# Turning both heads' queries at once with DMA copies between partitions, TensorE fillers, and weight splits moved one pair earlier

## The reference

```python
q_pool = q.reshape(B, H, S // 2, 2, D).mean(axis=3)          # B 4, H 8, S 1152, D 64
scores = scale * np.matmul(q_pool, k.transpose(0, 1, 3, 2))
scores = scores - np.max(scores, axis=-1, keepdims=True)
attn = np.exp(scores)
attn = attn / (np.sum(attn, axis=-1, keepdims=True) + 1e-09)
x = np.matmul(attn, v)                                        # then reshaped to 2304 x 512
...
h = x @ w_in                                                  # 512 x 1024
...
x = (ln @ w_out)                                              # 1024 x 512
...
for e in range(E):
    h = np.maximum(x[mask] @ w1[e], 0.0)
    out[mask] = gate_w[mask, None] * (h @ w2[e])
```

## Time and profile before

| | |
|---|---|
| median of three runs | 1127.13 us (1125.83 to 1127.24) |
| the profiled execution | 1129.12 us, of which its span is 1127.4 us |
| TensorE busy in the span | 1088.0 us (97%), 6647 instructions |
| VectorE busy | 750.0 us (67%) |
| ScalarE busy | 612.9 us (54%) |
| GpSimd busy | 381.5 us (34%) |
| attention | about 0 to 553 us |
| dense stage and routing | about 554 to 790 us |

### The profile page before, as it was taken

One profiled execution on the slowest core, in us unless ns is written; L12 is line 12 of the kernel. 1 busy time (PEld: TensorE's weight loads), 2 busy tenths in 40 slices (PEclk: granted clock), 3 DMA queues, 4 the chain that ended last, 5 costly groups with the idle time before them and its releaser, 6 DMA issues.

```text
span 1127.4 us, 20403 instructions
## 1 busy us (share of the span) xinstructions
PE 1088.0 (97%) x6647; PEld 767.4 (68%) x6647; DVE 750.0 (67%) x1632; ACT 612.9 (54%) x1327; POOL 381.5 (34%) x454
## 2 busy tenths in 40 slices
PE   7899999999999999999899999997989999999996
PEld 4565665556656565655588888886768888888885
DVE  4777787777778777777548999898775633333110
ACT  5676666667666666665465434435356534343221
POOL 4545544454554445445322211215112211111101
PEclk8899999999999999999899999999999999999998
DMA  4221122212112221102520000004556653311100
GB/s 129 64 60 36 53 64 64 62 47 56 44 48 65 64 64 46 40 21 77 150 85 19 28 20 19 28 30 185 171 180 239 228 182 113 106 38 49 39 21 1
DMA packets 92705, 85.59 MB, mean 76 GB/s; under 512 B 49006, under 2 KB 69486, under 8 KB 92464
## 3 DMA queue, kind: packets, MB, share of 16 engines
q1 hardware_dynamic: 88592, 72.92, 21.0%
q0 software_dynamic: 4000, 11.28, 3.1%
HBM read 74.73 MB, written 11.27 MB: 76 GB/s over the span
## 4 chain that ended last, share of the span: by engine, by line
PE 44%; DVE 2%; issue 2%; POOL 1%; ACT 1%; DMA 1%; DVEq 0%; ACTq 0%; POOLq 0%
PE h_ps L694 8%; PE h_ps L696 8%; PE h_ps L695 8%; PE o_ps L694 5%; PE o_ps L696 5%; PE o_ps L695 5%; PE t_ps L1170 2%; PE t_ps L1062 1%; PE h_ps L1137 1%; PE h_ps L1186 1%; DVE junk L1266 1%; DMA w_raw_e<-in_moe_w 1%; DVE w_split L1480 0%; POOL x_lo L973 0%; PE h_ps L1084 0%
## 5 line engine op out<-in xcount | busy, mean ns | idle before, releaser
L346 POOL TENSOR_SCALAR probs<-probs,scales 128x576 f32<-128x576 f32 x288 | 209.8, 748 | 263.6 <-DVE scales L547 263.6
L642 ACT ACTIVATE probs<-s_ps,lows 128x576 f32<-128x576 f32 x288 | 211.0, 737 | 146.5 <-DVE lows L518 146.1
L518 DVE TENSOR_REDUCE lows<-s_ps 128x1 f32<-128x576 f32 x288 | 205.2, 753 | 59.1 <-PE s_ps L423 51.3
L371 PEld LDWEIGHTS t_ps<-ident,probs 128*128 128x128 f32 x1152 | 123.8, 141 | 108.4 <-issue 100.4
L423 PE MATMUL s_ps<-kt,qt 64*128 64x288 f32 x1024 | 163.9, 438 | 4.8 <-ACT probs L642 4.8
L371 PE MATMUL t_ps<-ident,probs 128*128 128x128 f32 x1152 | 158.8, 281 | 2.8 <-POOL probs L346 2.0
L472 PE MATMUL pv_ps<-pt,values 128*64 128x512 f32 x576 | 155.2, 618 | 1.0 <-DVE x_t L582 1.0
L556 DVE COPY pt<-t_ps 128x512 f32<-128x512 f32 x144 | 99.4, 690 | 43.7 <-PE t_ps L371 43.6
L423 PEld LDWEIGHTS s_ps<-kt,qt 64*128 64x128 f32 x1024 | 89.3, 190 | 43.4 <-issue 24.5
L992 POOL DMA_INDIRECT out<-junk,target_rows x25 | 29.5, 1182 | 261.0 <-ACT junk L1699 260.7
L637 ACT COPY pt<-t_ps 128x512 f32<-128x512 f32 x144 | 84.4, 586 | 28.5 <-PE t_ps L371 24.5
(11 more groups left out here) (257 smaller groups left out, 2056.2 us busy)
## 6 DMA issues: line engine op xcount, KB each, us to landing
w_raw_e<-in_moe_w SPq DMA_DIRECT2D x60, 512.0 KB, 5.5
k_raw<-in_k SPq DMA_DIRECT2D x32, 256.0 KB, 2.8
q_raw<-in_q SPq DMA_DIRECT2D x32, 256.0 KB, 3.2
token_rows<-x_rows SPq DMA_DIRECT2D x18, 256.0 KB, 2.0
values<-in_v SPq DMA_DIRECT2D x32, 128.0 KB, 2.7
values<-in_v SPq DMA_DIRECT2D x64, 64.0 KB, 2.7
w_raw<-in_moe_w_in SPq DMA_DIRECT2D x4, 512.0 KB, 5.0
w_raw<-in_moe_w_out SPq DMA_DIRECT2D x4, 512.0 KB, 3.8
```

The lines of the kernel that those rows point to most:

```text
L346: nc.gpsimd.tensor_scalar(where, where, scales[:, g % 2, s, c:c + 1], 1.0, ALU.mult, ALU.mult).then_inc(norm_done if c else half_scaled, 1)
L371: last = nc.tensor.transpose(bank[:, i * P:(i + 1) * P], source, ident[:])
L518: nc.vector.tensor_reduce(lows[:, g % 2, s, c:c + 1], s_ps[c][:, :, 0:part], AX.XY, ALU.max, negate=True).then_inc(low_done[c], 1)
L642: nc.scalar.activation(two_halves(probs[g % 2][:, s, :])[:, :, columns(c)], s_ps[c][:, :, 0:part], ACT.Exp, bias=lows[:, g % 2, s, c:c + 1 ...
```

## The change

1. From pair 1 on, GpSimd adds the queries of both heads in one instruction, without `twice`; one turning (piece Q, slot 1) gives both heads, head 0 in partitions 0 to 63 of `qx` and head 1 in 64 to 127; four DMAs copy each half of `qx` into both halves of `qt`. The visit of slot 7 is gone.
2. In step 0 the pieces of pair 1 move from slots 0, 1, 2, 6, 7 to slots 4 to 7. SP loads the keys ahead of the values, and the queries of pair `at + 2` behind the copies.
3. Filler transposes of the identity stand behind every slot of step 0, at the end of attention and at the start of the dense stage; the ones at the program's start change their shapes.
4. `w_in` is loaded in step 14 and its high parts are made in slots 1, 2, 6, 7 of step 15; `w_out`'s are made in slots 4 to 7 of step 16. GpSimd's low parts of `w_in` may start once pair 14 is turned.
5. In slot 1 of step 16 the product stands between the two halves of the turning. The third batch's `merge_scales` of step 0 stands behind slot 8's maxima.
6. The first `x_lo` is made by VectorE (`first_x_lo`).

```diff
-    kq_slots = {0: KA, 1: QA, 2: TAILS, 6: KB, 7: QB}
+    kq_slots = {0: KA, 1: Q, 2: TAILS, 6: KB}
+    first_kq_slots = {4: KA, 5: Q, 6: TAILS, 7: KB}
+    high_slots = (1, 2, 6, 7)
...
+            def move_queries(n):
+                sp.wait_ge(kq_out, kq_count(n, Q))
+                for h in range(2):
+                    first = h * (full + 1)
+                    for u in range(2):
+                        sp.dma_start(qt[n % 2][rows(u), first:first + full, :].rearrange("p t n -> p (t n)"),
+                                     qx[rows(h), :]).then_inc(q_moved, 16)
...
             for at in range(pairs + 1):
+                n = at + 2
+                if n < pairs:
+                    sp.wait_ge(kq_done, kq_count(n - 1, KA))
+                    load_a(n)
                 if at < pairs:
                     if at >= 2:
                         sp.wait_ge(pv_done, key_tiles * (at - 1))
                     load_values(at)
-                n = at + 2
+                if at + 1 < pairs:
+                    move_queries(at + 1)
                 if n < pairs:
-                    sp.wait_ge(kq_done, kq_count(n - 1, KA))
-                    load_a(n)
-                    sp.wait_ge(q_sums, sum_count(n - 1, QA))
-                    load_qa(n)
+                    sp.wait_ge(q_sums, sum_count(n - 1, Q))
+                    load_q(n, 0)
+                    load_q(n, 1)
...
-            add_queries(0, 1)
-            add_queries(1, 0)
+            add_first_queries()
+            add_queries(1)
             add_tail(1)
             for g in range(pairs):
-                if g + 1 < pairs:
-                    add_queries(g + 1, 1)
                 normalise(g, 0)
                 if g + 2 < pairs:
-                    add_queries(g + 2, 0)
+                    add_queries(g + 2)
                     add_tail(g + 2)
                 for b in range(1, len(batches)):
                     normalise(g, b)
+            pool.wait_ge(t_done[1], key_tiles * (pairs - 1))
...
-            for i in range(18):
-                nc.tensor.transpose(s_ps[1][:, 1, 0:P], ident[:], ident[:])
-            for piece, bank in ((KA, t_ps[0]), (QA, t_ps[1]), (TAILS, third_ps)):
+            def warm(bank, times):
+                for i in range(times):
+                    nc.tensor.transpose(bank[:, 0:P], ident[:], ident[:])
...
+            warm(pv_ps, 3)
+            warm_halves(8)
+            warm(pv_ps, 2)
+            warm_quarters(4)
+            warm(pv_ps, 4)
...
+                        warm(pv_ps, 4 if s < 2 or has_kq(at, s) else 8)
                         continue
                     if i is not None:
                         turn_tiles(i, 0)
+                        if at == pairs and s == 1:
+                            multiply(m)
                         turn_tiles(i, 1)
...
+            warm(s_ps[0][:, 0, :], 8)
...
-                    if at == pairs and s > 0:
-                        c = s - 1
+                    if at == pairs - 1 and s in high_slots or at == pairs and in_chunks <= s < w_chunks:
+                        c = s if at == pairs else high_slots.index(s)
...
-                pe.wait_ge(x_lo_done, m + 1)
+                if m == 0:
+                    pe.wait_ge(first_x_lo, 1)
+                else:
+                    pe.wait_ge(x_lo_done, m)
...
+            for i in range(12):
+                nc.tensor.transpose(o_ps[:, 0:P], ident[:], ident[:])
...
+            dve.wait_ge(x_hi_done, 1)
+            nc.vector.tensor_tensor(x_lo[:, 0, :].rearrange("p (b n) -> p b n", n=P), columns_of(x_t, 0),
+                                    x_hi[:, 0, :].rearrange("p (b n) -> p b n", n=P).bitcast(F32),
+                                    ALU.subtract).then_inc(first_x_lo, 1)
```

More of the change, by code:

```diff
@@ L96, in build_attention @@
         k_tail = in_arena("k_tail", [P, 2, dim])
-        q_raw = [in_arena(f"q_raw{h}", [P, full, 2 * dim]) for h in range(2)]
+        q_raw = in_arena("q_raw", [P, full, 2, 2 * dim])
         q_tail = in_arena("q_tail", [P, 2 * dim])
-        q_sum = [in_arena(f"q_sum{h}", [P, full, 2, dim]) for h in range(2)]
+        q_sum = in_arena("q_sum", [P, full, 2, dim])
+        first_q_sum = in_arena("first_q_sum", [P, full, 2, dim])
+        kt_size = 2 * half
         kt = [in_arena(f"kt{i}", [P, 2, half]) for i in range(2)]
@@ L173, in has_kq, with kq_piece @@
         def has_kq(at, s):
-            return s in kq_slots and at + 1 < pairs
+            return s in (kq_slots if at else first_kq_slots) and at + 1 < pairs
+        def kq_piece(at, s):
+            return (kq_slots if at else first_kq_slots)[s]
         def has_rest(at, s):
@@ L304, in _ @@
                     load_b(n)
[L305 to L307 removed]
+                if at == pairs - 2:
                     for c in range(stages):
@@ L382, in kq_blocks @@
                     return [merged(k_tail[:]), merged(tail_sum[:])]
-                return [merged(q_sum[piece == QB][:, t, :, :]) for t in range(full)]
+                source = first_q_sum if piece == FIRST_QB else q_sum
+                return [merged(source[:, t, :, :]) for t in range(full)]
             def raw_ready(n, piece):
@@ L485, in multiply_rest, with warm_halves, warm_quarters @@
                 last.then_inc(pv_rest_done, 1)
-            for i in range(18):
-                nc.tensor.transpose(s_ps[1][:, 1, 0:P], ident[:], ident[:])
-            for piece, bank in ((KA, t_ps[0]), (QA, t_ps[1]), (TAILS, third_ps)):
+            def warm(bank, times):
+                for i in range(times):
+                    nc.tensor.transpose(bank[:, 0:P], ident[:], ident[:])
+            def warm_halves(times):
+                for i in range(times):
+                    for u in range(2):
+                        nc.tensor.transpose(s_ps[1][:, u, 0:dim], ident[rows(u), :], ident[rows(u), rows(u)])
+            def warm_quarters(times):
+                for i in range(times):
+                    for u in range(2):
+                        for h in range(2):
+                            nc.tensor.matmul(s_ps[1][rows(h), u, 0:dim], ident[rows(u), rows(h)],
+                                             ident[rows(u), rows(u)], start=True, stop=True)
+            warm(pv_ps, 3)
[3 more added lines that the diff above has]
+            warm(pv_ps, 4)
+            for piece, bank in ((KA, t_ps[0]), (FIRST_QA, t_ps[1]), (TAILS, third_ps)):
                 raw_ready(0, piece)
@@ L507, in _ @@
                         score_tile(at, s, at)
-                    if m is not None:
+                    if m is not None and not (at == pairs and s == 1):
                         multiply(m)
@@ L584, in _ @@
                         copy_rest(at, s)
-                    if s == 8 and at < pairs:
+                    if s == slots - 1 and 0 < at < pairs:
                         merge_scales(at, 2)
@@ L594, in _ @@
                                 merge_lows(at, b)
-                            if s == end and b < 2:
+                            if s == end and (b < 2 or at == 0):
                                 merge_scales(at, b)
@@ L622, in copy_kq @@
                 else:
-                    first = 0 if piece == QA else full + 1
+                    first = 0 if piece == FIRST_QA else full + 1
                     last = scaled(qt[par][:, first:first + full, :].rearrange("p t n -> p (t n)"), bank[:])
@@ L627, in next_kq @@
             def next_kq(g, s):
-                act.wait_ge(kq_done, kq_count(g + 1, kq_slots[s]))
-                copy_kq(1 - g % 2, kq_slots[s], third_ps, kq_out)
+                act.wait_ge(kq_done, kq_count(g + 1, kq_piece(g, s)))
+                if kq_piece(g, s) == Q and g > 0:
+                    act.wait_ge(q_moved, 64 * g)
+                copy_kq(1 - g % 2, kq_piece(g, s), third_ps, kq_out)
             def copy_turned(i):
```

81 lines of the change are left out of this document (45 added, 36 removed).

## The result

The change makes the kernel slower by a quarter of a per cent: 1129.27 us in the median (15 executions, 1127.63 to 1129.75) against 1126.32 (15, 1123.10 to 1129.16), a ratio of 1.0025 with a 95% interval of 1.0016 to 1.0034. The forecast was 1124.6, in a range up to 1128.8. Yet the two profiled executions stand the other way round: a span of 1125.9 us after, of 1127.4 before. The profiled execution of before took 1129.12, 2.8 above the median of its kernel; that of after was the shortest of 15. Both halves of this have to be explained: what the change costs, and what a single trace hid.

What follows compares the result with a forecast made beforehand. TensorE, busy 97% of the span, was taken as the bound outside some waits. Steady -0.5, first pair +3.9, step 16 -2.3, end fillers +0.1, dense start -1.0, clock -2.7 made -2.5: 1124.6 us from 1127.13, range 1117.5 to 1128.8.

Steps and rivals of the forecast that it cites:

- The first pair, +3.9: First pair: queries land later behind SP's queue, GpSimd normalises late and TensorE waits until 42.6: 3.9 us lost (+1.6 to +7).
- the clock, "+0.2": First pair: the low clock behind TensorE's wait costs about what it did, up to 2 us more: +0.2 us.
- The sum's base: Whole kernel: the summed gain of 2.5 us was taken from the median 1127.13, giving 1124.6 us.
- The 2.7 us of clock at the dense stage: Dense stage, tile 0's products: fillers keep the clock up, -2.7 us, or 0 if it falls anyway.
- Steady steps: Steps 1 to 14: slot 0's keys wait 0.40 us for ScalarE's copy `x_t`; 0.04 us gained each, -0.5 in all.
- step 16: Step 16: the product fills one wait and high parts made earlier remove others: -2.3 us (-1 to -2.7).
- rest product to first dense product: End of attention to dense stage: VectorE's earlier `x_lo` gives -1.0 us, the eight fillers cost +0.1.
- E: Rival, SP's queue: copies holding SP over 1.7 us each delay the queries every step; 1141 us at 1.9; chance 0.09.
- B: Rival, steady pairs: `x_t` moves too, so the removed visit's full worth arrives, 5.7 less: 1118.9 us; chance 0.17.
- C: Rival, first pair: GpSimd is not late and TensorE reaches step 1 some 4 us sooner: 1116.7 us; chance 0.06.
- D: Rival: fillers don't hold the clock; 2.7 of the dense stage lost, first pair 0.9 dearer: 1128.2 us; chance 0.13.

Runs made afterwards that it cites:

- The kernel with the sums behind: The changed kernel with GpSimd's sums for pair 2 (queries and tails) behind all normalisations of pair 0: 1121.49 us, ratio to before 0.9953.
- Fillers alone: The kernel before with 24 filler transposes in the wait at the dense stage's start and nothing else: 1125.41 us, ratio 0.9987.

## Why the prediction was wrong

**The first pair, +3.9, is the step that failed.** Its mechanism was right: SP's queue is behind, GpSimd stands before the load, TensorE before GpSimd. Its size was not. Over all profiles with the same code up to there, the rest product starts at 67.58, 66.19, 65.19, 65.58 and 65.08 before, 65.9 in the mean, and at 72.93, 73.43 and 71.69 after, 72.7: **+6.8 us**.

It has two parts. The last probabilities came to TensorE at 38.5 in the mean before (37.89 to 39.17) and at 44.0 after (43.82 to 44.40), 5.6 later where I had 3.4 (and 0.3 apart for a later start, which these 5.6 contain). Of the 2.2 that are missing, 0.7 is that my one trace of before was the latest of five; the rest is the list of GpSimd. `q_sum` started at 32.39 for the forecast's 32.1, with copies of 0.63 for 0.57. Then I let GpSimd add the tails at once; but SP issues their loads behind those of the queries, and GpSimd waited 1.08 us for them behind the sum, so the probabilities came at 43.89 for 42.6.

The second part is the clock, "+0.2". From the last wait to the rest product it takes 26.9 us at the upper level (65.19 - 38.34, and the same in two more), 28.3 and 28.4 in the two other profiles of before, and 29.0, 29.0 and 27.9 after: +1.2 in the mean. Before, the low stretch lay mostly over slots in which TensorE waited for ScalarE, and in three of five executions it was over by step 1; after, it lay in all three over step 1, where TensorE is the bound. The kernel with the sums behind brings the rest product back to 65.12, so the whole cost can be taken back by the order of GpSimd's list. What it takes back is the first part: the last probabilities come at 36.63, and from there it still takes 28.5 us, 0.57 of them a wait for `q_sum`, with a clock of 0.83 and 0.82 in the mean from 35 to 40 and from 40 to 45 us.

**The sum's base.** "It is 2.0 above the median; from 1127.13 the forecast is 1124.6" carried gains read from one long execution over to the median. The 2.7 us of clock at the dense stage were 2.45 in that trace, and about 1.1 in the mean of the five profiles without fillers. Fillers alone were worth 1.5 by the ratio (0.2 to 2.7). This is the second failed step, and the row of the clock in it was real: it was the execution that was not typical.

**What held.** Steady steps -0.04 each with a wait of 0.21 and the weight load, for the reason given; step 16 -2.18 for -2.3; rest product to first dense product -1.03 for -0.9 (`x_lo` and the eight fillers together); the copies are no rival (0.63 us of SP each, under the 1.7 from which E would have begun). Set up again with what executions in general show: +6.8, steps -0.5, step 15 +0.1, step 16 -2.2, dense start -1.0, clock -1.1, together **+2.1 us**. Measured are +2.95 and +1.9 by the medians of two comparisons, 1.1 to 3.8 by the two intervals.

**Rivals.** B (the visit's full worth) did not arrive, but was there to be had: with one copy moved on ScalarE the period is 0.41 under that of before, of 0.44. C (GpSimd not late) would not have given 4 us: with GpSimd in time the rest product starts at 65.1, 0.8 before the mean. D (fillers don't hold the clock) is out at the dense stage: twelve profiles with them at the upper level, three of five without at the lower one for a time. The Trainium skill, page "TensorE: Matmul & The Clock Gate", Part 4 on the PE-mode transpose, says that the upper clock doesn't come on for transposes in that mode, since they don't count as busy in the same way. The fillers are transposes of the program, though no row shows in which mode they run; the trace doesn't agree with the rule here (207.38 to 207.42 us in all twelve, up to 209.84 without).

**Open.** What decides in one execution whether the clock falls behind a wait of 2.45 to 3.65 us is not known; neither is why the first pair's rest product moves by up to 2.5 us between executions of the same code. Behind 766 us the lead of the changed kernel's profile grows from 0.7 to 2.1 us (797 us), over the routing stage, and is 1.5 at the end; I have not followed that. Nor was each part of the change run by itself: step 16's -2.2 and step 15's +0.1 are read from traces alone.

## What to carry over

Before a gain is taken from a trace, ask whether it is in every execution: compare the profiled execution's time with the median, and treat a low clock behind a short wait as an event with a chance. When a load is moved to the end of a queue, follow each item in the list of the engine that waits for it to the next one; moving one of two loads gave 0.5 us, which isn't clear of the noise; moving the work that waited for both gave 7.5. When TensorE is given less to do, look which engine's order now holds the resource it reaches too soon: one short copy, put ahead of one short exponential, let nearly the whole worth of the removed visit arrive (0.41 of 0.44 us a step).

## What the runs showed of the hardware

Behind a wait of about the same length at the dense stage's start, without fillers, TensorE ran at the lower level for a time in three profiles (waits of 3.65, 3.64 and 2.45 us) and not in two (3.64 and 2.45), two of these five being of one and the same kernel. Where it fell, it fell at different moments: within the wait of 3.65 us (the granted clock was 0.64 in the mean over the last 2 us ahead of the first product, which then took 0.79), or only under the second product behind the wait of 2.45 us (0.50, 0.56, 0.63 us in the rows above). With transposes of 128 by 128 in that wait it was at the upper level in all twelve profiles; ahead of a wait of 6 us they brought nothing that is clear of the noise. A copy between partitions of 128 KB, issued by SP as one instruction with rows of 2 KB, held its queue for 0.63 us (2.52 for four), as long as a load of values from memory (0.60 to 0.63); a load of keys of 256 KB held it for 0.34. VectorE's `below`, of two or four columns, ended with GpSimd's instruction in the changed kernel (336.91 and 336.89) as it did before (327.71 and 327.70).
